# Dense layers on six batches of finished tokens, with tokens as weights in the second layer, and straight code for eight experts

## What is computed

```python
# attention: 4 batches x 8 heads x 576 tokens, window 128, linear bias -> x [2304, 512]
# experts (N=2304 tokens, D=512, E=8 experts, F=1024): each token belongs to one expert
logits = x @ w_gate; cap = N // E                      # 288
for idx in argsort(-logits.flatten()):                 # best (token, expert) pairs first
    if token is free and counts[e] < cap: assign it
for e in range(E):
    h = maximum(x[mask_e] @ w1[e], 0); out[mask_e] = h @ w2[e]
# dense layers (512 -> 2048 -> 512) on all tokens
h = out @ w_in; g = h * sigmoid(h); return g @ w_out
```

## Time and profile before

| | |
|---|---|
| time, median of 3 runs | 933.9 us (933.51 to 934.63) |
| profiled execution, its own time | 934.12 us |
| span of that execution | 932.4 us |
| TensorE matmuls busy | 882.0 us, 95% of the span, 7532 instructions |
| VectorE busy | 498.2 us, 53% |
| ScalarE busy | 370.7 us, 40% |
| GpSimd busy | 299.2 us, 32% |
| granted TensorE clock, mean | 0.973 |
| DMA | 70.89 MB, mean 76 GB/s |

### The profile page before, as it was taken

The page is one execution under the profiler, slowest core; times in us unless marked ns, Lnnn a source line. Parts: engine busy times, 40 slices in busy tenths (PEclk is TensorE's granted clock), DMA queues, the critical chain, the costliest instruction groups (busy, mean ns, idle before and its releaser), DMA issues.

```text
span 932.4 us, 20957 instructions
## 1 busy us (share of the span) xinstructions
PE 882.0 (95%) x7532; PEld 860.7 (92%) x7532; DVE 498.2 (53%) x1635; ACT 370.7 (40%) x880; POOL 299.2 (32%) x302
## 2 busy tenths in 40 slices
PE   7999999932999999999999999999999999999995
PEld 6999999922999999999999999999999999999995
DVE  6666666568655555555645555555556545642210
ACT  5666656502333433443244234333432433244322
POOL 1332222413124323513361325135223604261322
PEclk9999999965999999999999999999999999999998
DMA  6655666203303023111302130213113021203000
GB/s 161 149 148 148 153 155 163 91 14 116 89 4 108 28 71 98 43 53 48 105 25 77 38 99 17 90 46 94 34 56 115 25 67 48 90 25 92 27 1 26
DMA packets 117312, 70.89 MB, mean 76 GB/s; under 512 B 61712, under 2 KB 103696, under 8 KB 117264
## 3 DMA queue, kind: packets, MB, share of 16 engines
q1 hardware_dynamic: 114192, 60.85, 23.5%
q0 software_dynamic: 3072, 9.44, 3.4%
HBM read 60.83 MB, written 9.44 MB: 75 GB/s over the span
## 4 chain that ended last, share of the span: by engine, by line
PE 74%; DVE 3%; POOL 1%; ACT 1%; issue 0%; ACTq 0%; DVEq 0%
PE hp L962 12%; PE acc L962 12%; PE acc L964 11%; PE hp L964 11%; PE hp L963 11%; PE acc L963 11%; PE rt L913 3%; PE tp L957 1%; PE rt L932 1%; PE tp L947 1%; DVE wa_l L1291 1%; DVE test L1143 1%; PE rt L917 1%; POOL out_dram L866 1%; DVE test L1258 0%
## 5 line engine op out<-in xcount | busy, mean ns | idle before, releaser
L885 POOL TENSOR_TENSOR h_l<-gate,h_h 128x288 fp32r<-128x288 f32 x128 | 104.7, 819 | 222.9 <-ACT h_h L1094 222.7
L874 POOL TENSOR_TENSOR wb_l<-wb_raw,wb_h 128x512 fp32r<-128x512 f32 x64 | 87.1, 1363 | 227.0 <-ACT wb_h L1045 226.7
L962 PE MATMUL hp<-y_h,res_h 128*128 128x288 f32 x512 | 155.5, 304 | 0.0
L962 PE MATMUL acc<-h_h,res_h 128*128 128x288 f32 x512 | 154.5, 302 | 0.3 <-POOL h_l L885 0.3
L963 PE MATMUL hp<-y_l,res_h 128*128 128x288 f32 x512 | 151.0, 295 | 0.0
L964 PE MATMUL acc<-h_h,res_l 128*128 128x288 f32 x512 | 150.8, 295 | 0.0
L964 PE MATMUL hp<-y_h,res_l 128*128 128x288 f32 x512 | 150.7, 294 | 0.0
L963 PE MATMUL acc<-h_l,res_h 128*128 128x288 f32 x512 | 150.1, 293 | 0.0
L1316 DVE TENSOR_TENSOR gate<-hp,gate 128x288 f32<-128x288 f32 x128 | 58.4, 456 | 142.4 <-ACT gate L1082 142.4
L1082 ACT ACTIVATE gate<-hp 128x288 f32<-128x288 f32 x128 | 52.6, 411 | 162.5 <-PE hp L964 155.5
L962 PEld LDWEIGHTS acc<-h_h,res_h 128*128 128x128 f32 x512 | 96.3, 188 | 0.7 <-POOL h_l L885 0.5
(11 more groups left out here) (208 smaller groups left out, 1873.3 us busy)
## 6 DMA issues: line engine op xcount, KB each, us to landing
wa_raw<-in_moe_w_dram SPq DMA_DIRECT2D x64, 256.0 KB, 2.6
wb_raw<-in_moe_w_dram SPq DMA_DIRECT2D x64, 256.0 KB, 2.8
q_rows<-in_q_dram SPq DMA_DIRECT2D x32, 128.0 KB, 3.3
k_rows<-in_k_dram SPq DMA_DIRECT2D x32, 128.0 KB, 2.7
v_rows<-in_v_dram SPq DMA_DIRECT2D x32, 128.0 KB, 2.4
stage<-in_moe_w_in_dram SPq DMA_DIRECT2D x8, 512.0 KB, 4.5
x_rows<-x_rows_sb SPq DMA_DIRECT2D x16, 256.0 KB, 3.9
stage<-in_moe_w_out_dram SPq DMA_DIRECT2D x8, 512.0 KB, 4.5
```

The source lines that it names most:

```text
L874: pool.tensor_tensor(wb_l[f % RING][:], wb_raw[f % RING][:], wb_h[f % RING][:].bitcast(FP32), ALU.subtract).then_inc(wb_low, 1)
L885: pool.tensor_tensor(h_l[f % 3][:], gate[f % 2][:], h_h[f % 3][:].bitcast(FP32), ALU.subtract).then_inc(g_low, 1)
L962: nc.tensor.matmul(out_, weights_h, cols_h, start=start, stop=False)
```

## The change

- **Stages.** The work becomes fourteen stages in the order of `STAGES`: "A" i is expert i's two layers (16 slots), "M" k is the dense layers on batch k (32 slots). A batch is a range of columns of one shared buffer `xy_h`, `xy_l` of 608 columns, into which each expert writes its 288 result columns at `X_COL`. The six batches have 256, 512, 384, 512, 256 and 384 tokens. Experts 1 and 2 follow each other without a dense stage between, and so do 4 and 5.
- **First dense layer** (`dense_a`): as before, but 256, 384 or 512 columns per matmul.
- **Second dense layer** (`dense_b`): 128 tokens of `h_h` or `h_l` are the weights, and the 512 output features of `res_h` or `res_l` are the columns. The result has tokens as rows, one bank per 128 tokens. `turn_result` and `yT` are gone; ScalarE and VectorE copy the banks to `rows` (`copy_out`), and GpSimd scatters 128 rows at a time.
- **Order.** The lag of a slot b in the dense stages is one tile instead of two (`M_LAG`): a0, a1, b0, a2, b1, .... Buffers for `h_h` and `h_l` are two halves of one tile of 1024 columns, and the product is written where `h_l` will stand.
- **Routing and splits.** `HOOK_LIST` gives each expert's sixteen parts their slots, counted over all 320 slots. Stages begin at slots 0 (A0), 16 (M0), 48 (A1), 64 (A2), 80 (M1), 112 (A3), 128 (M2), 160 (A4), 176 (A5), 192 (M3), 224 (A6), 240 (M4), 272 (A7) and 288 (M5).
- **Token lists.** A batch's list of tokens crosses experts, so each expert's `tokens` goes to DRAM by SP (`write_list`) and comes back 128 to a column (`read_list`).
- **Loops.** TensorE, ScalarE and VectorE run straight code for all eight experts.

```diff
+STAGES = [("A", 0), ("M", 0), ("A", 1), ("A", 2), ("M", 1), ("A", 3), ("M", 2), ("A", 4), ("A", 5), ("M", 3), ("A", 6),
+          ("M", 4), ("A", 7), ("M", 5)]
+X_COL = [320, 288, 0, 96, 320, 32, 96, 0]
+BATCH = [(320, 256), (96, 512), (0, 384), (96, 512), (32, 256), (0, 384)]
+A_LAG, M_LAG = 2, 1
-HOOK_AT = [3, 4, 6, 7, 9, 10, 12, 13, 16, 17, 19, 20, 22, 25, 29, 31]
-SETUP_AT = 0
-OUT_AT = [2, 4, 6, FT1 * 2]
-X_AT = [40, 42, 44, 46]
-FETCH_AT = [31, 33, 35]
+SETUP_AT = {0: 1, 32: 2, 82: 3, 114: 4, 140: 5, 180: 6, 226: 7}
+HOOK_LIST = {
+    1: [3, 4, 6, 7, 9, 10, 12, 13, 16, 17, 19, 20, 22, 25, 28, 29],
+    2: [34, 35, 37, 38, 40, 41, 43, 44, 46, 47, 49, 50, 51, 53, 55, 56],
+    3: [84, 85, 86, 87, 88, 89, 90, 91, 92, 93, 94, 95, 97, 99, 101, 102],
+    4: [116, 117, 119, 120, 122, 123, 125, 126, 128, 129, 131, 132, 134, 136, 138, 139],
+    5: [142, 143, 145, 146, 148, 149, 151, 152, 154, 155, 157, 158, 160, 162, 164, 165],
+    6: [182, 183, 185, 186, 188, 189, 192, 193, 195, 196, 198, 199, 201, 203, 205, 206],
+    7: [228, 229, 231, 232, 234, 235, 237, 238, 240, 241, 243, 244, 246, 248, 250, 251],
+}
...
+            def dense_b(s, k, f):
+
+                tiles = BATCH[k][1] // P
+                pe.wait_ge(g_low, FT2 * k + f + 1)
+                if f == 0:
+                    pe.wait_ge(y_low, (STAGES[s - 1][1] + 1) * DC)
+                o = FT2 * DM + DM * f
+                for t in range(tiles):
+                    m = slice(512 * (f % 2) + P * t, 512 * (f % 2) + P * (t + 1))
+                    nc.tensor.matmul(acc[t][:], h_h[:, m], res_h[:, o:o + DM], start=(f == 0), stop=False)
+                    nc.tensor.matmul(acc[t][:], h_h[:, m], res_l[:, o:o + DM], start=False, stop=False)
+                    last = nc.tensor.matmul(acc[t][:], h_l[:, m], res_h[:, o:o + DM], start=False, stop=(f == FT2 - 1))
+                    if f == FT2 - 1 and t < tiles - 1:
+                        last.then_inc(acc_done, 1)
+                last.then_inc(b_done, 1)
...
+                        if FT2 * i + f > 0:
+                            act.wait_ge(g_done, FT2 * i + f)
+                        nc.scalar.activation(gate[:, 0:width], hp[(A_NO[s, f] - 1) % 2][:, 0:width], ACT.Sigmoid
+                                             ).then_inc(sig_done, 1)
+                for w in SPLIT_A.get(n, []):
+                    high_a(w)
+                for w in SPLIT_B.get(n, []):
+                    high_b(w)
+                if kind == "a" and stage == "M":
+                    act.wait_ge(g_done, FT2 * i + f + 1)
+                    nc.scalar.activation(h_h[:, h_cols(s, f)], h_raw[:, h_cols(s, f)], ACT.Copy
+                                         ).then_inc(g_high, 1)
```

More of the change, by code:

```diff
@@ L1029, in _ @@
                 turn_x(0, c, acc[c])
-            with pe.Fori(0, E - 1) as i:
-                body(i, True)
-            body(E - 1, False)
-            for c in range(DC):
-                turn_result(E, c, last_banks[c])
+            for n, (s, kind, f) in enumerate(SLOTS):
+                if n in HOOK_AT:
+                    part(*HOOK_AT[n])
+                for j, c in X_AT.get(n, []):
+                    turn_x(j, c, x_bank(j, c))
+                stage, i = STAGES[s]
+                if stage == "A":
+                    (expert_a if kind == "a" else expert_b)(s, i, f)
+                else:
+                    (dense_a if kind == "a" else dense_b)(s, i, f)
@@ new lines, in copy_out @@
+            def copy_out(s, k):
+                tiles = BATCH[k][1] // P
+                for t in range(1, tiles, 2):
+                    if t < tiles - 1:
+                        dve.wait_ge(acc_done, acc_before(s, t) - s)
+                    else:
+                        dve.wait_ge(b_done, B_NO[s, FT2 - 1])
+                    if k + 1 < len(BATCH):
+                        dve.wait_ge(xt_done, DC * (STAGES[s + 1][1] + 1))
+                    if k > 0:
+                        dve.wait_ge(scattered, 16 * TILES_OUT[k])
+                    nc.vector.tensor_copy(rows[:, t, :], acc[t][:]).then_inc(out_odd, 1)
```

541 lines of the change are left out of this document (286 added, 255 removed).

## The result

| | before | changed |
|---|---|---|
| median | 933.7 us (933.03 to 934.63) | **985.3 us** (983.7 to 988.5) |
| ratio | | 1.0556, interval 1.0525 to 1.0586 |
| span of the profiled execution | 932.4 us | 984.7 us |
| granted TensorE clock, mean | 0.973 | 0.949 |

The change costs 5.6%. The forecast was 939.5 us, and its range ended at 958: it had the right side, slower, and the wrong size.

A forecast was written before the change was run, and what follows sets the result against it. It took TensorE's matmul stream as the bound. From 934.1 us it took 28.8 us of savings and added 34 us of new waits: 939.3, rounded to 939.5 us, with an 8-in-10 range of 921 to 958.

The forecast's parts named there:

- The token list, "nothing": Token list through DRAM on SP: costs nothing, as SP is behind only weight loads with a ring of four.
- The falling clock: Rival: TensorE's clock drops in the five new gaps of over 2 us, costing 10 us: 949 us, chance 0.10.
- Pitch: Dense layers: time between starts of large matmuls; fewer, wider matmuls gain 13.7 us, with 226 ns at 512 columns.
- reading (a): Dense layers: the extra 13 ns come once per matmul, 226 ns at 512 columns, a gain of 13.7 us; taken.
- reading (c): Rival, dense layers: a slower rate per column, 236 ns at 512 columns, no gain: 953 us, chance 0.08.
- reading (b): Rival, dense layers: the extra 13 ns vanish in long streams, 382 us, a gain of 26: 927 us, chance 0.17.
- Waits on VectorE and GpSimd, +34: TensorE in the new slot order: waits summing to 39.4 us, less 5 for overlap, so +34 (18 to 40).
- position step to list: Routing: TensorE waits before the list matmuls, now two slots behind the position matmuls (three for expert 1): 11.5 us.
- preference step to first count: Routing: VectorE's 3.3 us step now has two slots instead of three, behind other work; TensorE waits 7.4 us.
- other steps: Routing: the closing-expert step gets two slots and the step behind the list one; TensorE waits 7.6 us.
- h_l, and the rest: Dense stages' shorter lead, 7.4 us, plus mid-batch waits and a late token transpose, 5.5; 5 off for waits shortening others.
- Transposes and end: Expert loop and kernel end: dropping result transposes saves 10.6 us, a shorter chain after the last matmul 3.9 us.

The follow-up runs named there:

- late lists: Changed kernel with each token list written to DRAM only right before its batch's list is read, behind the stage's last weight tile: 967.1 us, ratio 1.0346.
- best version: Changed kernel with late lists, routing parts and preference steps re-placed, and second-layer products two slots behind the first in the 256-token batches: 932.0 us, ratio 0.9971.

## Why the prediction was wrong

Forecast 939.5, measured 985.3, 45.8 us more. By its own steps:

**The token list, "nothing"** (failed, 18.2 us). I said that SP is behind nothing but weight loads that have a ring of four. I asked whether SP waits, and not what its transfers do to those behind them. Two writes of 288 scattered numbers take 8.8 us to land and the 256 KB loads of wa around them 10.7 in the median, where the same loads in the same stage take 2.8 with late lists. The ring of four, one tile used every 3.2 us, does not cover that. The late lists return 18.2 us, and putting them back in the best version costs 18.1. This is the step that failed by most.

**The falling clock, a rival at 0.10 and 10 us** (failed as weighed, about 14 us). The mechanism was named, with its price for a stretch (2 us per wait; measured 1.4 to 1.5). The reason against it, "the gaps are short and stand in a full stream", was wrong: a wait of 3.1 us brings the stretch (experts 2, 4 and 7), and those of 1.8 and 2.3 us at the lists in A1 and A4 do too, though the one of 1.9 us in M4 does not. Forecasting 34 us of waits in a stream at full clock, it had to be a term of the sum. The 14 us are an estimate: 6.8 measured, and for the other 17 us of half clock 1.45 us for each 3.4. With late lists, so without what the list writes add, it is 34 us of half clock and by the same price 14.6 us.

**Pitch** (mis-sized, 7.8 us). 226 ns was forecast at 512 columns and 232 measured, reading (a) against (c) with 236. The excess over one column a cycle is 12.4, 13, 15 and 18.7 ns at 256, 288, 384 and 512 columns: a part that is fixed and a part that grows. Near reading (c), which I gave 0.08. I took the fixed cost from one width alone. The prediction named this sign of being wrong, a pitch off by more than 5 ns, and it is off by 6. Two of its side sums are also off: reading (b) makes 383 us and not 382, and the rule of the Trainium skill 374 and not 379. That rule (216 ns at 512 columns) is off by 16 ns here.

**Waits on VectorE and GpSimd, +34** (right in sum, partly by luck). Without what the list writes do, they are 32.4 us (lists late). Inside the sum one term came out at twice its size and two at about half and two thirds:

| term | forecast | measured |
|---|---|---|
| position step to list | 11.5 | 7.7 |
| preference step to first count | 7.4 | 14.6 |
| other steps | 7.6 | 3.9 |
| h_l, and the rest | 12.9 less 5 | 6.2 |

The preference step is the term that was put at half of what it is. Expert 6 was put at 0.8 us and is 3.35; experts 2, 4 and 7 at 1.9 to 2.3 and are 3.0 to 3.2. There are two causes. For experts 4 and 7 the step itself takes its 3.3 us, but it starts late: the weight remainder ahead of it on VectorE waits for ScalarE's rounding, and that for a load of 3 us. The chain of waits in front of the first count of expert 4, in the changed kernel:

```profile
503.42 3.05 DMA wa_raw<-in_moe_w_dram
506.50 0.64 ACT wa_h L1139
507.16 0.74 DVE wa_l L1382
```

VectorE stands idle for 1.4 us before that remainder, and for 1.5 at expert 7. The prediction counted the split's own time there and not this wait. For experts 2, 5 and 6 the step is longer. I had it at 3.3 us from the earlier trace rows, where GpSimd stood idle. Now it meets GpSimd's remainders. For expert 2 the conversion that takes 0.16 to 0.17 us elsewhere takes 1.24 until a GpSimd operation has ended, and the step 4.4 us:

```profile
303.02 1.24 DVE L1244 TENSOR_SCALAR half<-best 128x20 int32<-128x20 int32 x1
```

```profile
302.88 1.35 POOL L969 TENSOR_TENSOR wb_l<-wb_raw,wb_h 128x512 fp32r<-128x512 f32 x1
```

The Trainium skill ("SBUF — State Buffer", section "SBUF: two separate sides") says that VectorE in a two-port mode and GpSimd share a port pair as an exclusive lock, held for a whole instruction, and the one that comes second blocks. 303.02 + 1.24 is 304.26, and GpSimd's operation ends at 304.23; the trace agrees in time. In which mode this conversion ran, it doesn't tell.

The list waits of experts 2, 4, 5 and 7 stood where they were forecast (1.8, 1.4, 2.3, 1.9 us against 3.0, 1.7, 3.2, 2.7), that of expert 1 is 0.3 against 0.9, and there are none in the 512-token batches. The first second-layer slot of a batch waits 0.6 to 0.9 us against "about 1" and 0.7, but the long waits are in the batches of 256 and the short ones in those of 512, the other way round.

**Transposes and end** (each 1 us too much). The transposes give 9.6 us and not 10.6, since 0.33 us holds beside a routing group only. The end gives 2.8 and not 3.9: the prediction took TensorE's end at 919.33, where the first copy starts, and the stream ran to 920.3.

**Right**: unrolled code and gathers at nothing, since no wait on either shows behind the first.

What is left of the 45.8 us: 18.2 + 14.6 + 7.8 + 1.0 + 1.1 - 1.6 = 41.1, so about 5 us stay. The span of the best version leaves as much: 932.4 less the gains of 5.9, 9.6, 2.8 and 0.6, plus 10.5 of waits, is 924.0 against 928.9, at full clock in the loop, so it is neither clock nor lists. TensorE's timelines hold about 3 of them: the steps that are 0.05 us or more over the pitch with no wait in the view (at 512 columns the second matmul then follows after 0.32 us and not 0.23) cost 7.4 us in the kernel before and 10.6 in the best version, 114 instead of 84. The rest, about 2 us, is open; that TensorE stands a little longer at each wait than the view says is a candidate.

## What to carry to other kernels

A small DMA can be a slow one, and what it costs depends on what is queued behind it: put a scattered write of a few hundred numbers behind the urgent loads and gathers, not right in front of them. Where work of a second engine is released in slots of the first, write the distance of each step in microseconds of that slot kind; an order that fits slots of 133 ns x 12 and a lag of four does not fit other widths, and gains of 19 us turned into a loss of 52 here. When waits of 2 to 3 us are forecast in a dense stream, their half clock belongs in the sum, at 1.4 us for a stretch of 3.4 us here. Where a step of one engine stands behind work that waits for a load, count that wait too, and not only the work.

## What the hardware showed that I had not expected

- A list write, 1.1 KB in pieces of 4 bytes, took 7.7 us to land in the median of twelve, and loads of 256 KB behind two of them took 10.7 us instead of 2.8. A gather on GpSimd's own queue was held up as well (10.6 us against 4.9, and 12.75 in the kernel before with the writes added).
- The pitch of these fp32r matmuls is not one column a cycle plus a constant: 119, 133, 175 and 232 ns at 256, 288, 384 and 512 columns.
- Filling four holes of TensorE with products that nobody reads kept the clock at 1.00 behind all four, in one profiled execution. A wait of 3.1 us in an otherwise full stream was enough to lose it.
- VectorE's small operations on 20 numbers a row stretched from 0.17 to 1.0 and 1.24 us beside a GpSimd operation.
